# Second pair's units normalised and transposed ahead of layer 2, in the order in which their rows are mixed; four units' halves held in the tables' space

## What is computed

```python
num = einsum(phi(q), phi(k)^T v);  x = num / den           # linear attention, phi: 64 features per head
u  = x + real(fft(fft(x, axis=1), axis=2))                 # "mixed rows"
un = (u - mean(u)) / sqrt(var(u) + 1e-06)                  # over the 128 channels of a token
x2 = u + relu(un @ w_ch1) @ w_ch2                          # layer 1, hidden width 512
h  = relu(x2 @ w_in)                                       # layer 2, hidden width 1024
out = (h * sigmoid(conv3(h))) @ w_out                      # conv3: three taps along the sequence
```

## Time and profile before

| what | value |
| --- | --- |
| median of 3 runs | 263.29 us (262.94 to 263.55) |
| the profiled execution, whole | 263.48 us |
| its span (what the profile covers) | 261.7 us |
| PE, DVE, ACT, POOL busy in the span | 95%, 85%, 70%, 14% |
| granted TensorE clock, whole span | 1.00 |
| slots 14 to 22 on PE | 100.64 to 118.43 us of the span |
| layer 2 opening: hidden chunks 0 to 5 with slots 23 to 27 on PE | 118.43 to 138.87 us |

### The profile page before, as it was taken

The page is one execution under the profiler, slowest core; times in us unless marked ns, Lnnn a source line. Parts: engine busy times, 40 slices in busy tenths (PEclk is TensorE's granted clock), DMA queues, the critical chain, the costliest instruction groups (busy, mean ns, idle before and its releaser), DMA issues.

```text
span 261.7 us, 4307 instructions
## 1 busy us (share of the span) xinstructions
PE 249.6 (95%) x1524; PEld 211.2 (81%) x1524; DVE 221.2 (85%) x391; ACT 183.2 (70%) x354; POOL 36.4 (14%) x90
## 2 busy tenths in 40 slices
PE   8999999999999999999959999998999999999985
PEld 6999999889899999988847777786778677777753
DVE  0747877997998789889999989989959999998992
ACT  2341435423576546577998998999989989978872
POOL 0000000000703333138980000000000000000000
PEclk9999999999999999999999999999999999999999
DMA  6958830210000000000000000002000002002002
GB/s 199 361 233 314 324 93 3 54 44 0 3 0 3 1 1 3 0 1 4 0 0 3 0 0 0 0 4 85 0 0 3 0 0 85 5 0 85 0 0 85
DMA packets 4341, 13.04 MB, mean 50 GB/s; under 512 B 736, under 2 KB 1504, under 8 KB 4320
## 3 DMA queue, kind: packets, MB, share of 16 engines
q1 hardware_dynamic: 4320, 12.77, 13.4%
HBM read 10.54 MB, written 2.23 MB: 49 GB/s over the span
## 4 chain that ended last, share of the span: by engine, by line
PE 78%; DVE 14%; ACT 5%; issue 3%; DVEq 0%; ACTq 0%
PE ps L590 20%; PE ps L511 9%; PE ps L513 8%; PE ps L512 8%; PE ps L428 6%; PE ps L504 5%; PE ps L440 5%; PE ps L551 4%; PE ps L469 4%; PE ps L453 3%; DVE arena L1018 3%; DVE arena L1023 2%; PE ps L596 2%; ACT arena L783 1%; DVE arena L933 1%
## 5 line engine op out<-in xcount | busy, mean ns | idle before, releaser
L590 PE MATMUL ps<-arena,wout 128*128 128x364 f32 (+1 forms) x192 | 62.9, 468 | 0.7 <-DVE arena L1030 0.7
L590 PEld LDWEIGHTS ps<-arena,wout 128*128 128x128 f32 x192 | 35.8, 189 | 20.8 <-issue 2.8
L783 ACT ACTIVATE arena<-ps 128x364 f32<-128x364 f32 x96 | 40.6, 479 | 5.0 <-PE ps L513 4.4
L1018 DVE SCALAR_TENSOR_TENSOR arena<-arena,taps 128x1088 f32<-128x1088 f32 x32 | 43.2, 1351 | 0.8 <-ACT arena L791 0.6
L1023 DVE SCALAR_TENSOR_TENSOR arena<-arena,taps 128x1088 f32<-128x1088 f32 x32 | 43.2, 1351 | 0.1
L1030 DVE TENSOR_TENSOR arena<-arena 128x1088 f32<-128x1088 f32 (+2 forms) x36 | 41.5, 1163 | 1.6 <-ACT arena L796 1.5
L511 PE MATMUL ps<-x2hi,wlo 128*128 128x364 f32 x96 | 39.6, 412 | 0.8 <-ACT arena L783 0.6
L796 ACT ACTIVATE arena<-arena 128x1088 f32<-128x1088 f32 x32 | 35.5, 1111 | 1.9 <-DVE arena L1023 1.9
L791 ACT ACTIVATE arena<-arena,taps 128x1088 f32<-128x1088 f32 x29 | 35.1, 1210 | 0.6
L513 PE MATMUL ps<-x2hi,whi 128*128 128x364 f32 x96 | 31.5, 328 | 0.0
L512 PE MATMUL ps<-x2lo,whi 128*128 128x364 f32 x96 | 31.5, 328 | 0.0
(11 more groups left out here) (82 smaller groups left out, 432.5 us busy)
## 6 DMA issues: line engine op xcount, KB each, us to landing
arena<-v_d SPq DMA_DIRECT2D x4, 594.0 KB, 3.9
arena<-qT_d SPq DMA_DIRECT2D x3, 545.0 KB, 6.9
arena<-kT_d SPq DMA_DIRECT2D x3, 544.5 KB, 6.0
out_d<-arena SPq DMA_DIRECT2D x3, 544.0 KB, 2.7
cos_t<-cos_d SPq DMA_DIRECT2D x1, 926.5 KB, 5.7
sin_t<-sin_d SPq DMA_DIRECT2D x1, 926.5 KB, 7.5
arena<-qT_d SPq DMA_DIRECT2D x2, 272.5 KB, 4.4
wraw<-w_d SPq DMA_DIRECT2D x2, 256.0 KB, 5.1
```

Of the source, the lines that this page charges most:

```text
L590: pe.matmul(ps[:, OUT_BANK + t, 0:z - a], wout[:, c, :], gate[:, i % GATES, a:z], start=(c == 0), stop=(c == C2 - 1)).then_inc(wout_done, 1)
L783: act.activation(h2[:, i % HIDDENS, t * TT:(t + 1) * TT], ps[:, bank_p(n), 0:TT], ACT.Relu).then_inc(h2_ready, 1)
L1018: dve.scalar_tensor_tensor(out=gate[:, i % GATES, 1:S + 1], in0=h2[:, i % HIDDENS, 0:S], scalar=taps[:, i % C2, 0:1], in1=gate[:, i % GATE ...
```

## The change

- The units get an order of their own for getting ready, `TURN_ORDER`: 0 to 5, then 8, 6, 9, 7. Below, *place* p is the p-th unit in this order. The order in which slots use the units stays 0 to 9.
- `MOMENTS_AT` has place 6 in slot 14, place 7 in 17, place 8 in 18, place 9 in 20 (before: 6, 7, 8, 9 in slots 17, 20, 21, 22).
- `ROWS_AT` and `TURNS_AT` are new. `normed_rows` of places 5 to 8 in slots 15, 17, 19, 21; turns, highs and lows in slots 16, 18, 20, 22. Place 9 (unit 7) is normalised by ACT after `relu(0)`, turned by PE after `hidden(1)`, split by ACT after `relu(1)` and by DVE after `left_tap(0)`. No unit is turned later.
- Places 6 to 9 have a buffer each for their halves, `late_hi` and `late_lo`, in the space that `cos_t` and `sin_t` had; so their highs and lows wait for no earlier unit's use.
- Places 6 to 9 are turned into bank 5 in place of bank 2; place 5 stays in bank 1.

```diff
-ROWS_OF = [1 + max((b // BP) * NJ + j for _, b, j in unit) for unit in UNITS]
+TURN_ORDER = [0, 1, 2, 3, 4, 5, 8, 6, 9, 7]
+RING, LAST_TURN = 6, 1
+ROWS_OF = [1 + max((b // BP) * NJ + j for _, b, j in UNITS[unit]) for unit in TURN_ORDER]
-MOMENTS_AT = {1: 2, 5: 3, 9: 4, 13: 5, 17: 6, 20: 7, 21: 8, 22: 9}
+MOMENTS_AT = {1: 2, 5: 3, 9: 4, 13: 5, 14: 6, 17: 7, 18: 8, 20: 9}
+ROWS_AT = {0: 1, 4: 2, 8: 3, 12: 4, 15: 5, 17: 6, 19: 7, 21: 8}
+TURNS_AT = {2: 1, 6: 2, 10: 3, 14: 4, 16: 5, 18: 6, 20: 7, 22: 8}
...
-        cos_t = sb("cos_t", [128, TABLES, TQ])
-        sin_t = sb("sin_t", [128, TABLES, TQ])
+        with ExitStack() as tables:
+            cos_t, sin_t = (tables.enter_context(nc.sbuf_tensor(name, [128, TABLES, TQ], F32)) for name in ("cos_t", "sin_t"))
+        late_hi = sb("late_hi", [128, NR - RING, G1], F32R)
+        late_lo = sb("late_lo", [128, NR - RING, G1], F32R)
+        spare_tables = sb("spare_tables", [128, 2 * (TABLES * TQ - (NR - RING) * G1)])
...
-        def bank_turned(r):
-            return 1 if r <= NJ else 2
+        def bank_turned(place):
+            return 1 if place < RING else 5
...
+        def turned(place):
+            return (unhi[:, place % 2, :], unlo[:, place % 2, :]) if place < RING else (late_hi[:, place - RING, :], late_lo[:, place - RING, :])
...
                 if c == 0:
-                    pe.wait_ge(unhi_ready, r + 1)
-                    pe.wait_ge(unlo_ready, r + 1)
+                    pe.wait_ge(unhi_ready, TURN_ORDER.index(r) + 1)
+                    pe.wait_ge(unlo_ready, TURN_ORDER.index(r) + 1)
...
-                if c == 2 and n < FIRST_SLOTS:
-                    normed_transposes(r + 1)
+                if n in TURNS_AT:
+                    normed_transposes(TURNS_AT[n])
...
-                for r in turns_at(2 * i):
-                    normed_transposes(r)
+                if i == LAST_TURN:
+                    normed_transposes(NR - 1)
...
-                if c == 0 and r + 1 < NR:
-                    normed_rows(r + 1)
+                if n in ROWS_AT:
+                    normed_rows(ROWS_AT[n])
...
             relu(0)
+            normed_rows(NR - 1)
...
-                if c == 2 and r < NJ:
-                    normed_low(r + 1)
+                if n in TURNS_AT:
+                    normed_low(TURNS_AT[n])
```

More of the change, by code:

```diff
@@ L304, in token_views @@
                            x2[:, b0, first:first + step * 2 * TQ:step].rearrange("p (t j) -> p t j", j=2))
-        def turns_at(place):
-            first = max(FIRST_SLOTS, slots_before(place - 1)) if place else FIRST_SLOTS
-            return [n // C1 + 1 for n in range(first, slots_before(place)) if n % C1 == 2 and n // C1 + 1 < NR]
         def slots_a(i):
@@ L533, in up @@
                 three_pass(ps[:, bank_h1(n), 0:G1], whi[:, c * 128:(c + 1) * 128], wlo[:, c * 128:(c + 1) * 128],
-                           unhi[:, r % 2, :], unlo[:, r % 2, :], True, True).then_inc(w1_done, 1)
+                           *turned(TURN_ORDER.index(r)), True, True).then_inc(w1_done, 1)
             def down(n):
@@ L646, in _ @@
                     project(n)
-                for r in turns_at(2 * i + 1):
-                    normed_transposes(r)
                 for n in slots_b(i):
@@ L712, in normed_rows @@
                     act.wait_ge(ut_done, r)
-                for m, u in enumerate(normalised(r)):
+                for m, u in enumerate(normalised(TURN_ORDER[r])):
                     act.activation(un[:, m, :], u, ACT.Identity,
@@ L718, in normed_high @@
                 act.wait_ge(ut_done, r + 1)
-                if r >= 2:
+                if 2 <= r < RING:
                     act.wait_ge(w1_done, C1 * (r - 1))
-                act.activation(unhi[:, r % 2, :], ps[:, bank_turned(r), 0:G1], ACT.Copy).then_inc(unhi_ready, 1)
+                act.activation(turned(r)[0], ps[:, bank_turned(r), 0:G1], ACT.Copy).then_inc(unhi_ready, 1)
             def hidden_high(n):
@@ L744, in slot @@
                     mixed_high(r - 1)
-                if c == 2 and n < FIRST_SLOTS:
-                    normed_high(r + 1)
+                if n in TURNS_AT:
+                    normed_high(TURNS_AT[n])
             act.wait_ge(ones_ready, 1)
@@ L815, in _ @@
                     relu(i + 1)
-                    for r in turns_at(2 * i + 2):
-                        normed_high(r)
+                    if i + 1 == LAST_TURN:
+                        normed_high(NR - 1)
                     for n in slots_a(i + 1):
@@ L821, in _ @@
                         middle_tap(i + 1)
-                    for r in turns_at(2 * i + 3):
-                        normed_high(r)
                     for n in slots_b(i + 1):
@@ L943, in normed_low @@
                 dve.wait_ge(unhi_ready, r + 1)
-                if r >= 2:
+                if 2 <= r < RING:
                     dve.wait_ge(w1_done, C1 * (r - 1))
-                dve.tensor_tensor(unlo[:, r % 2, :], ps[:, bank_turned(r), 0:G1], unhi[:, r % 2, :].bitcast(F32),
+                high, low = turned(r)
+                dve.tensor_tensor(low, ps[:, bank_turned(r), 0:G1], high.bitcast(F32),
                                   ALU.subtract).then_inc(unlo_ready, 1)
@@ L968, in slot @@
                     mixed_low(r - 1)
-                if c == 2 and r == NJ:
-                    normed_low(r + 1)
                 if n in MOMENTS_AT:
@@ L1040, in _ @@
                     left_tap(i)
-                for r in turns_at(2 * i + 2):
-                    normed_low(r)
+                if i + 1 == LAST_TURN:
+                    normed_low(NR - 1)
                 for n in slots_a(i + 1):
```

## The result

The changed kernel takes 261.94 us (median of 10 runs, 261.18 to 262.34) against 263.13 for the kernel before on the same chip (10 runs): ratio 0.9953, 95% interval 0.994 to 0.9967, so 1.2 us less (0.9 to 1.6). Run once more beside other experiments it gave 0.993 (0.9913 to 0.9947). The profiled execution took 261.73 us with a span of 259.9, where the one of before had 263.48 and 261.7.

What follows compares the result with a forecast made beforehand. PE, busy 95% of the span, was taken as the bound, with DVE and ACT bounding layer 2's opening. +0.65 at hidden(6) and -2.57 late gave -1.9 us, from 263.29 to 261.4 us; range 259.3 to 263.8.

Steps and rivals of the forecast that it cites:

- Front, +3.0: Slots 14 to 22: added turns and waits start hidden(0) at 121.4 in place of 118.43, +3.0 us.
- Opening, +0.65 at hidden(6): hidden(0) to hidden(6): vanished waits pay 2.35 of the 3.0 us, so hidden(6) comes only 0.65 us later.
- PE's three waits around unit 7's turn: Opening of layer 2: PE waits of 0.77, 1.27 and 1.89 us were taken out of its 20.44 us.
- The step that says what holds hidden(6): Opening: DVE's chain ends right_tap(2) at 137.85, then sigmoid(2) at 137.95, relu(5), and hidden(6) at 139.5.
- Late part, -2.57: Chunks 10 to 15: the turns of units 8 and 9 leave with their waits, -2.57 us.
- A reason beside it: Late part: ACT loses 3.9 us of work, so relu(15) should come ahead of PE and the whole term counts.
- the second rival: Opening: the front's shift stays whole because DVE or ACT needs as long as before; +0.4, 263.7 us, chance 0.15.
- The third: Opening: place 9's GpSimd chain runs under the taps, hidden(6) +4.2; +2.3, 265.6 us, chance 0.08.
- list of edits taken at nothing: Whole kernel: halves' new place, bank 5, vanished w1_done waits and unchanged DMA were counted as costing and gaining nothing.

Runs made afterwards that it cites:

- a2: The changed kernel with moments of place 6 in slot 15 in place of slot 14, behind unit 4's low half; 0.9889 of the kernel before.
- a3: The changed kernel with unit 4's x2hi ahead of place 8's normed_rows in ACT's slot 21; 0.9889 of the kernel before.
- a4: The changed kernel with both edits of a2 and a3; 0.9892 of the kernel before.
- c1: a4 with place 7's moments in slot 16 in place of 17; 0.9937 of the kernel before.
- a1: The kernel before with only units 6 and 7 turned into bank 5, nothing moved; 0.9925 of the kernel before.
- c2: a3 with place 9's turn behind hidden(4) in place of hidden(1); 0.9918 of the kernel before.
- b2: The changed kernel with two blank PE turns into bank 2, at chunks 10 and 15, read by nobody; 0.9993 of the kernel before.
- b3: The changed kernel with place 9's moments behind left_tap(0) on DVE in place of slot 20; 1.0241 of the kernel before.
- d1: c3 with moments of place 6 in slot 15, those of place 9 in slot 21 and its rows behind relu(1); 259.51 us, 0.9865 of the kernel before.
- b1: The changed kernel with places 6 to 9 turned into bank 2 in place of bank 5; 1.0103 of the kernel before.
- c3: c2 with the middle tap of chunk 3 moved from ACT to DVE; 0.9886 of the kernel before.

## Why the prediction was right, and where it wasn't

The forecast was 261.4 us, -1.9 us, range 259.3 to 263.8. Measured 261.94, -1.2 us (0.9 to 1.6), and -1.8 in the repeat; by the mark -1.6. Sign and places were right, and the size within 0.7 us; the working can be laid beside the trace term by term.

**Front, +3.0.** By the mark +3.3. Each wait came at its place: up(16) 1.17 later by the mark (forecast 1.20), the turn in slot 20 with a wait of 0.70 (0.95), hidden(0) behind place 8's rows, x2hi and x2lo. The term is 0.3 too small, and its last step accounts for that. x2lo ended at 121.03 and hidden(0) started 0.51 us later, not 0.1 as I had taken. The rows of before already had 0.36: x2lo ends at 118.07, hidden(0) starts at 118.43. The repeat has 0.36 too; why it is 0.36 in some profiles and 0.51 in others was not tried. a2 and a3 show that both causes cost, and a4 and c1 that they stand in line: whichever is taken away, the next in the row of moments, chain, rows and turn holds hidden(0), so that each alone, and both together, give 0.5 to 0.6 us.

**Opening, +0.65 at hidden(6).** By the mark +0.88 (38.43 against 37.55). DVE's wait for place 9's high was 1.21 (1.5), right_tap(2) ended at 137.8 (137.85), sigmoid(2) started at 138.00 (137.95), hidden(6) at 139.54 (139.5). On the scale of before, on which the forecast stands, the measured ones are 0.21 later, as hidden(0) is; the stretch itself took 18.00 (18.1). That PE's three waits around unit 7's turn would be gone is shown by a1, which takes away nothing else. The step that says what holds hidden(6) named only DVE's chain; the profile and c2 show that ACT held it to within 0.2 us of the same time. That the number came out with one of the two left out is partly luck.

**Late part, -2.57.** From hidden(6) to the down of slot 35 it took 46.59 us before (185.46 - 138.87) and 44.14 after (183.68 in the chain of work, less 139.54), so -2.45. The sum was right, its parts less so: from the end of the down at 174 us to the next but one it took 8.91 us, where the forecast had PE's own 8.61 (so 1.79 won there, forecast 2.09), and 0.65 was won ahead of it (0.48). A reason beside it was wrong: relu(15) did not come ahead of PE, it ran at 180.74 as before (180.71), because ACT waits for PE at 174.8 and is full from there. It was enough that nothing of layer 1's turns waits in bank 2 behind slot 34 any more. b2 shows it: with a blank turn in that place the 1.0 us is back.

**Rivals.** None came. The shift of the front does pass whole into hidden(6) where bank 2 is out of play (18.0 us in eight of the profiles), so the second rival's mechanism is there; the gain from bank 2 (2.44 us of the opening) was on top of it. The third did not come, and its price was not measured. b3 makes the moments late, but its chain ran beside an idle DVE and took 2.8 us; it shows that moments that late cost more than the rival's 4.2 us without any slow chain. d1 has the end of the chain under the taps (4.4 us), but nothing waits for it. On the Trainium skill's rule on shared SBUF interfaces (page "GPSIMD Engine Reference", section "8. Key points"): all five chains from slot 13 on took 2.8 to 3.0 us here, against 8.8 under the taps before, which agrees with it, as does the end of the chain in d1.

**What the forecast lacked** is the share of each part. Its list of edits taken at nothing has bank 5, with only its next user in mind; b1 puts its price at 4.2 us. By the mark the change gives 1.6 us; the bank alone, for two units, gives 1.4 (a1), and the moving in bank 2 loses 2.6 (b1). Moving all turns to the front costs 3.3 us there and takes 2.45 out of the late part; with bank 5 it is worth its cost only because it frees the late part as well, where bank 5 is not to be had. What the new order and the four buffers of their own give by themselves was not taken apart.

## What to carry to other kernels

Before moving work to avoid a wait, look in which buffer the wait is: two producers of different pace that share one PSUM bank cost here as much as the whole move won, and one line took it away. When work is moved ahead of a stage, follow each in-order queue by its slots; the first instruction that had no slack (here a low half with 0.1 us) tells what is lost. And a wait taken away in a row of dependent steps shows only up to the next one: test edits together before adding their gains.

## What the runs showed of the hardware

**The clock after an idle.** In b3, PE stood idle for 5.95 us, up to 131.45. The granted clock, 1.00 in the profiles of all other kernels from 100 to 200 us, was 0.50 from 128 to 134 us, and the matmuls of 436 columns started 0.37 us apart (132.62, 132.99) where they start 0.20 apart at 1.00. It cost 1.5 us on top of the wait. In the profile of b1 a wait of 2.24 us left the clock at 1.00; three other executions of b1 had a mean of 0.986 to 0.994, and no trace shows at which place.

**A shift from the start.** Profiles of kernels with the same first 14 slots differ in where the mark lies by up to 1.6 us: 100.34 us in c3 and 101.90 in a1. For these two the difference is there from the start. Busy time of PE from 5 to 7 us of the span, in a1 and then in c3 (the first column in brackets is the number of matmuls):

```profile
5.00:7.00 2.00, 2.00 (x10) 1.78 (x9) 0.00 (x0) 0.00 (x0) 0.00 (x0) 1.00 0.93 276
```

```profile
5.00:7.00 2.00, 2.00 (x23) 2.00 (x21) 0.00 (x0) 0.54 (x2) 0.00 (x0) 1.00 0.97 295
```

In the one, 10 matmuls were listed in 2 us, in the other 23, with a granted clock of 1.00 listed in both and 14 in the kernel before. The count alone doesn't give the shift: the changed kernel had 16 and in its repeat 19, but the repeat then waited 0.43 us for a DMA at 9.71, and the mark lay at 101.11 and 101.10. What lets PE go faster sooner was not tried, and, with one or two profiles of each kernel, neither was whether the shift belongs to the execution or to the kernel. It can be as large as this change's effect, so a difference of two spans can't be read without taking it out.
